# Up-projection operands: made once per pair of tiles, stored to memory and loaded back in two later blocks

## The chip, the cores and the metric

The program runs on one core of a Trainium2 chip. The metric is the device time of one execution in microseconds (us), as a median over runs. The engines are TensorE (PE; its weight loads are listed as PEld), VectorE (DVE), ScalarE (ACT), GpSimd (POOL) and SyncE (SP); each works through its own instruction queue in order and waits on semaphores. Here SP's queue issues nearly all transfers between memory and the on-chip buffers.

## The reference

```python
# attention with decay, per head; state is 64 x 64
state = gamma * state + k_t v_t^T ;  y_t = scale * q_t state
x = y as (3072 tokens, 512)

# first feed-forward layer: 512 -> 2048 -> 512
h = x @ w_in
g = where(h > 0, h, exp(min(h, 0)) - 1)
x = g @ w_out

# second layer: 512 -> 1024 -> 512
h = x @ w_in2 ;  e = exp(h - max(h)) ;  solu = h * e / (sum(e) + 1e-9)
ln = (solu - mean) / sqrt(var + 1e-6) * g_ln
out = ln @ w_out2
```

Every matmul operand is split into a high part, in the format fp32r that PE multiplies, and a low part, the rest (value minus high part). A product is three matmuls: high by high, low by high, high by low.

## The kernel before

There are three stages: attention (to about 82 us of the trace), the first feed-forward layer (to about 570 us), the second layer. The change is in the first layer.

**Blocks and units.** The 3072 tokens are cut in three blocks (`NBLK`) of 1024, and each block in two halves of 512. The 2048 hidden columns are taken 256 at a time: eight units a block (`NFP = 8`), 24 in all (`NU`), numbered n. Unit n of a block multiplies two tiles of `w_in` with both halves of x at once, by Winograd's form of Strassen's product, which needs seven products instead of eight. For that the 2 x 2 arrangement of the weights (A11, A12, A22 and the fourth quadrant, which is loaded into the slot S1) needs four sums (S1 to S4), and x needs four (T1 to T4). The seven left operands, S1 to S4 and three quadrants, each 128 x 256, are the "up operands" of the unit. They depend on the weights and on n % 8, not on the block.

**How the up operands are made.** Two ring slots, n % 2, hold them. Each slot has a high buffer `u_hi` and a low buffer `u_lo`, 7168 bytes a partition each; `u_raw` is another name for the bytes of `u_lo`. For every unit of every block:

- SP, `load_u(n)`: waits until unit n-2 has done its product M4, then loads 512 KB of `w_in` into four of the seven places of `u_raw`.
- POOL, `sum_u(n, i)`, four instructions (L483).
- ACT, `split_u_hi(n)`, one instruction on all seven (L1096), which waits for the fourth sum. It stands in ACT's queue in the middle of `quadrants(n-1)`, ahead of the exponentials of that unit's last three quadrants and ahead of the copy of the next unit's first product (`p1_kept`, L1159).
- POOL, `split_u_lo(n, i)`, seven instructions (L488).
- PE, `up(n, ...)`, lines 618 to 620: waits for `ul_done`, the count of low parts.

**A unit on PE.** `up_pair` runs the products in the order M1, M6, M2, M7, M5, then a `down` product (12 matmuls, L665, L666, L669) of the unit before, then M4 and M3, then the first `down` of this unit: 42 + 24 = 66 matmuls. M2 adds to the bank in which M1 stands, so PE waits for ACT's copy of M1 (`p1_kept`) ahead of it. ACT and DVE make the four quadrants of the hidden values in `quadrants(n)`, with ELU as Relu, Exp and a maximum, and split them into `g_hi` and `g_lo`. After the eight units the second half's 16 `down` products run, in which the next block's x is prepared: DVE's queue holds `sum_x` and `split_x_lo` between its `split_g_lo` instructions (L878), and ACT's queue `split_x_hi` between its `split_g_hi`. The first `sum_x` (L841) stands behind the low split of f = 3 and the evacuation (L884), and ahead of the low split of f = 4; it waits for `load_x`, 2048 KB (L353), which SP issues after product M3 of the block's last unit.

**SP's order around the change.** Attention's loads and the stores of its outputs come first, then 14 loads of `w_out` tiles (`load_wd`, 256 KB each, L364), then the loop over the blocks with `load_u`, the stores of x2 and `load_x`.

The order is written out by hand in each engine's program; no scheduler moves anything.

Of the kernel before, what the change touches and what calls it, by code (L numbers as in the profile page):

```python
# [7 lines left out]
P = 128  # L8
# [18 lines left out]
NFP = NF1 // 2  # L27
NU = NBLK * NFP
# [19 lines left out]
TILE_OF = {place_of(n): n for n in range(NCH)}  # L48


def build(nc, units, w1, w_in2, w_out2, g_ln, tables, x_dram, x2_dram, out):
    f32, f32r = mybir.dt.float32, mybir.dt.float32r
    ALU, ACT, AX = mybir.AluOpType, mybir.ActivationFunctionType, mybir.AxisListType

# [1 line left out]
    with ctx:  # L56
# [8 lines left out]
        def place(name, cols, dt, at):  # L65
            return nc.alloc_sbuf_tensor_at(name, [P, cols], dt, offset=at)
# [40 lines left out]
        u_hi = [place(f"u_hi{s}", 7 * 256, f32r, RING_AT + 14336 * s)[:, :].rearrange("p (o c) -> p o c", c=256)  # L107
                for s in range(2)]
        u_lo = [place(f"u_lo{s}", 7 * 256, f32r, RING_AT + 14336 * s + 7168)[:, :].rearrange("p (o c) -> p o c", c=256)
                for s in range(2)]  # L110
# [89 lines left out]
        def up_bank(blk):  # L200
            return 4 * (blk % 2)
# [11 lines left out]
        def sem(name):  # L213
            return ctx.enter_context(nc.semaphore(name))
# [25 lines left out]
        xh_done = sem("xh_done")  # L240
        xl_done = sem("xl_done")
        u_raw_in = [sem(f"u_raw_in{s}") for s in range(2)]
        u_summed = sem("u_summed")
        uh_done = sem("uh_done")
        ul_done = sem("ul_done")
# [3 lines left out]
        part_done = sem("part_done")  # L249
# [38 lines left out]
        M1, M6, M2, M7, M5, M4, M3 = range(1, 8)  # L288
# [3 lines left out]
        LEFT = [A11, S2, A12, S3, S1, A22, S4]  # L292
# [3 lines left out]
        def products(u, i):  # L296
            return 7 * u + i
# [4 lines left out]
        def quads(n, i):  # L302
            return 4 * n + i

        def after(order, slot):
            return order.index(slot) + 1
# [14 lines left out]
        def _(sp):  # L321
# [29 lines left out]
            def load_x(blk):  # L351
                sp.wait_ge(part_done, products(NFP * blk - 1, M3))
                sp.dma_start(x_raw[:, 0:4, :, :].rearrange("p o k t -> p (o k t)"),  # L353
                             x_dram[blk - 1].rearrange("p h k t -> p (h k t)")).then_inc(x_raw_in, 16)

            def load_u(n):
                if n >= 2:
                    sp.wait_ge(part_done, products(n - 2, M4))
                i = n % NFP
                sp.dma_start(u_raw[n % 2][:, 0:4, :].rearrange("p o c -> p (o c)"),  # L360
                             w1[:, 2 * i:2 * i + 2, :].rearrange("p f c -> p (f c)")).then_inc(u_raw_in[n % 2], 16)

# [3 lines left out]
            def store_x2(blk, half):  # L366
                done = 2 * (2 * blk + half + 1)
                sp.wait_ge(x2_act, done)
                sp.wait_ge(x2_dve, done)
                for i in range(CB):  # L370
                    sp.dma_start(x2_dram[TILE_OF[blk, half, i], :, :].rearrange("p (k t) -> p k t", k=KD),
                                 x2[half][:, :, i * C:(i + 1) * C]).then_inc(x2_stored[half], 16)
# [34 lines left out]
            for blk in range(NBLK):  # L407
                for i in range(NFP):
                    if i == 0 and blk > 0:
                        store_x2(blk - 1, 1)  # L410
                    if NFP * blk + i + 2 < NU:
                        load_u(NFP * blk + i + 2)
                if blk == 0:
                    for s in range(CB, NS):
                        sp.wait_ge(x_stored[s], 32)
                    sp.dma_start(gln_sb[:, :], g_ln).then_inc(gln_in, 16)
                    sp.dma_start(ident[:, :], tables[:, T_IDENT:T_IDENT + P]).then_inc(gln_in, 16)
                if blk < NBLK - 1:
                    load_x(blk + 1)
                    store_x2(blk, 0)  # L420
# [31 lines left out]
        def _(pool):  # L452
# [19 lines left out]
            def sum_u(n, i):  # L472

                raw = u_raw[n % 2]
                to, a, b, op = ((S3, A11, S1, ALU.subtract), (S1, S1, A22, ALU.add),
                                (S2, S1, A11, ALU.subtract), (S4, A12, S2, ALU.subtract))[i]
                if i == 0:
                    pool.wait_ge(u_raw_in[n % 2], 16 * (n // 2 + 1))
                else:
                    pool.wait_ge(u_summed, 4 * n + i)  # L480
                if n >= 2 and to == S4:
                    pool.wait_ge(part_done, products(n - 2, M3))
                nc.gpsimd.tensor_tensor(raw[:, to, :], raw[:, a, :], raw[:, b, :], op).then_inc(u_summed, 1)  # L483

            def split_u_lo(n, i):
                o = LEFT[i]
                pool.wait_ge(uh_done, n + 1)
                nc.gpsimd.tensor_tensor(u_lo[n % 2][:, o, :], u_raw[n % 2][:, o, :], u_hi[n % 2][:, o, :].bitcast(f32),  # L488
                                        ALU.subtract).then_inc(ul_done, 1)
# [3 lines left out]
            for s in range(NS):  # L493
# [6 lines left out]
                if s >= 8:  # L500
                    split_u_lo(0, 2 * (s - 8))
                    if s < NS - 1:
                        split_u_lo(0, 2 * (s - 8) + 1)
            for n in range(1, NU):
                for i in range(4):
                    sum_u(n, i)
                for i in range(7):
                    split_u_lo(n, i)
# [44 lines left out]
        def _(pe):  # L553
# [55 lines left out]

            def up(n, i, bank, a, b, first):  # L610
                blk = n // NFP
                pe.wait_ge(ul_done, products(n, after(LEFT, a)))
                if n % NFP == 0:
                    pe.wait_ge(xl_done, products(blk, after(RIGHT, b)))
                for k in range(2):
                    one = slice(k * P, (k + 1) * P)
                    hi, lo = u_hi[n % 2][:, a, one], u_lo[n % 2][:, a, one]
                    nc.tensor.matmul(bank, hi, x_hi[:, b, k, :], start=(first and k == 0), stop=False, skip_group_check=True)  # L618
                    nc.tensor.matmul(bank, lo, x_hi[:, b, k, :], start=False, stop=False, skip_group_check=True)  # L619
                    done = nc.tensor.matmul(bank, hi, x_lo[:, b, k, :], start=False, stop=(k == 1), skip_group_check=True)  # L620
                done.then_inc(part_done, 1)
# [95 lines left out]
            for blk in range(NBLK):  # L717
                for i in range(NFP):
                    n = NFP * blk + i
# [343 lines left out]
        def _(act):  # L1063
# [61 lines left out]
            def exponent(n, i, h):  # L1125

                z = quads(n, i)
                if z > 3:

                    act.wait_ge(g_done, z - 3)  # L1130
                    if i in (G22, G12):
                        act.wait_ge(gl_done, down_no((n - (i == G22)) // NFP, 0, 2 * ((n - (i == G22)) % NFP) + (i == G22)) + 1)
                one = e[:, (z - 1) % 3, :]
                nc.scalar.activation(one, h, ACT.Relu, scale=-1.0).then_inc(r_done, 1)
                act.wait_ge(r_done, z)
                nc.scalar.activation(one, one, ACT.Exp, scale=-1.0).then_inc(e_done, 1)
# [15 lines left out]
            def quadrants(n):  # L1152
                blk, i = n // NFP, n % NFP
                X = ps[:, up_bank(blk), :]
                e11, e21 = (e[:, (quads(n, q) - 1) % 3, :] for q in (G11, G21))
                act.wait_ge(part_done, products(n, M1))
                if n >= 2:
                    act.wait_ge(g_done, quads(n - 2, G21))
                nc.scalar.activation(p1[:, n % 2, :], X, ACT.Copy).then_inc(p1_kept, 1)  # L1159
                act.wait_ge(part_done, products(n, M2))  # L1160
                exponent(n, G11, X)
                if blk == 0 and i > 0:
                    wd_split_hi(2 * i)
                act.wait_ge(g_done, quads(n, G11))
                split_g_hi(down_no(blk, 0, 2 * i), e11)
                if n + 1 < NU:
                    split_u_hi(n + 1)
                if i == 0 and blk > 0:
                    evacuate(blk - 1, 1)
                if blk == 0 and i > 0:  # L1170
                    wd_split_hi(2 * i + 1)
                act.wait_ge(h_summed, sums(n, H22))
                exponent(n, G22, stash[:, 2 * i + 1, :])
                if i == NFP - 1:
                    split_g_hi(down_no(blk, 1, 0), stash[:, 0, :])
                act.wait_ge(h_summed, sums(n, H21))
                exponent(n, G21, p1[:, n % 2, :])
                act.wait_ge(g_done, quads(n, G21))
                split_g_hi(down_no(blk, 0, 2 * i + 1), e21)
                act.wait_ge(h_summed, sums(n, H12))  # L1180
                exponent(n, G12, stash[:, 2 * i, :])
# [151 lines left out]
```

## Time and profile before

| what | value |
|---|---|
| median of 3 runs | 854.62 us (853.29 to 854.78) |
| profiled execution, own time | 853.04 us |
| its span, first to last instruction | 851.2 us |
| busy: PE / DVE / ACT / POOL | 98% / 64% / 49% / 46% |
| granted TensorE clock, mean | 0.998 |
| memory traffic | 56.50 MB read, 16.78 MB written |
| attention stage ends, unit 0 begins | 82.16 us |

PE's busy share counts pipelined matmuls, whose shown durations (389 ns) overlap; how densely PE works is read from how many matmuls start in a stretch. The other engines' shares are averages over stages. A row of a timeline gives start, duration, engine, line, operation, output and inputs, and in square brackets how long the engine had been idle and what ended that. Rows of SPq are issues of transfers, not the transfers.

### The profile page before, as it was taken

To read this page: it belongs to the slowest core of one execution; us is meant where nothing else is said; L and a number is where in the kernel's file an instruction comes from. 1 tells how busy PE (TensorE), PEld (TensorE's weight loads), DVE (VectorE), ACT (ScalarE), POOL (GpSimd) and SP (SyncE) were. 2 spreads that over 40 slices of the span, in tenths; PEclk is the share of its full clock that TensorE was granted. 3 is DMA by queue.
4 is the path that set the end of the run, shared out by engine and by line. 5 is a ranking of instruction groups with operands and counts; after the bars stand their busy time and mean duration, and the time that the engine had idled before them with its cause. 6 is when DMAs were issued, how large, how long until landed. Compare 5 with 4: busy or idle time off the path is not lost.

```text
span 851.2 us, 12588 instructions
## 1 busy us (share of the span) xinstructions
PE 834.4 (98%) x4850; PEld 691.7 (81%) x4850; DVE 548.3 (64%) x846; ACT 418.5 (49%) x678; POOL 389.2 (46%) x446
## 2 busy tenths in 40 slices
PE   7999999999999999999999999999999999999998
PEld 5888788888888888888888888877888888888886
DVE  2587676768635554575455455787888777777773
ACT  3696656565535555544455554563334333334432
POOL 2669575764016576620267560374253343444200
PEclk9999999999999999999999999999999999999999
DMA  9999610104003010140201002513011111111001
GB/s 348 404 377 313 211 50 25 50 25 170 8 0 99 26 49 26 29 170 1 74 25 50 25 25 87 161 50 99 26 50 50 50 50 38 50 50 50 25 13 50
DMA packets 49643, 74.10 MB, mean 87 GB/s; under 512 B 3248, under 2 KB 23984, under 8 KB 49328
## 3 DMA queue, kind: packets, MB, share of 16 engines
q1 hardware_dynamic: 49152, 73.22, 25.4%
q8 instruction: 39, 0.64, 0.3%
q14 instruction: 20, 0.16, 0.1%
q10 hardware_dynamic: 432, 0.07, 0.0%
HBM read 56.50 MB, written 16.78 MB: 86 GB/s over the span
## 4 chain that ended last, share of the span: by engine, by line
PE 89%; DVE 5%; ACT 2%; POOL 2%; DMA 1%; issue 1%; SPq 0%; DVEq 0%; ACTq 0%
PE ps L665 9%; PE ps L666 9%; PE ps L669 9%; PE ps L618 9%; PE ps L620 9%; PE ps L619 9%; PE ps L766 5%; PE ps L768 5%; PE ps L767 5%; PE ps L677 4%; PE ps L679 4%; PE ps L678 4%; PE ps L595 3%; PE ps L752 2%; PE ps L570 2%; PE ps L583 1%
## 5 line engine op out<-in xcount | busy, mean ns | idle before, releaser
L488 POOL TENSOR_TENSOR u_lo<-u_raw,u_hi 128x256 fp32r<-128x256 f32 x168 | 142.0, 878 | 194.6 <-ACT u_hi L1096 194.6
L665 PE MATMUL ps<-g_hi,wd_hi 128*128 128x512 f32 x384 | 149.4, 389 | 0.0
L666 PE MATMUL ps<-g_hi,wd_lo 128*128 128x512 f32 x384 | 149.4, 389 | 0.0
L669 PE MATMUL ps<-g_lo,wd_hi 128*128 128x512 f32 x384 | 149.4, 389 | 0.0
L618 PE MATMUL ps<-x_hi,u_hi 128*128 128x512 f32 x336 | 131.3, 391 | 0.8 <-ACT p L1159 0.8
L620 PE MATMUL ps<-x_lo,u_hi 128*128 128x512 f32 x336 | 130.8, 389 | 0.0
L619 PE MATMUL ps<-x_hi,u_lo 128*128 128x512 f32 x336 | 130.7, 389 | 0.0
L483 POOL TENSOR_TENSOR u_raw<-u_raw 128x256 f32<-128x256 f32 x96 | 88.0, 917 | 18.0 <-DMA u_raw<-w_dram 12.5
L669 PEld LDWEIGHTS ps<-g_lo,wd_hi 128*128 128x128 f32 x384 | 72.1, 188 | 15.0
L665 PEld LDWEIGHTS ps<-g_hi,wd_hi 128*128 128x128 f32 x384 | 72.1, 188 | 15.0
L666 PEld LDWEIGHTS ps<-g_hi,wd_lo 128*128 128x128 f32 x384 | 72.1, 188 | 14.9
L527 POOL TENSOR_TENSOR u_lo<-x_raw,u_hi 128x256 fp32r<-128x256 f32 x84 | 65.9, 823 | 23.2 <-ACT u_hi L1207 23.2
L766 PE MATMUL ps<-wd_hi,n_hi 128*128 128x512 f32 x192 | 75.8, 395 | 0.0
L618 PEld LDWEIGHTS ps<-x_hi,u_hi 128*128 128x128 f32 x336 | 63.0, 188 | 15.4 <-ACT p L1159 1.9
L768 PE MATMUL ps<-wd_hi,n_lo 128*128 128x512 f32 x192 | 74.8, 389 | 0.0
L767 PE MATMUL ps<-wd_lo,n_hi 128*128 128x512 f32 x192 | 74.8, 389 | 0.0
L620 PEld LDWEIGHTS ps<-x_lo,u_hi 128*128 128x128 f32 x336 | 63.1, 188 | 13.2
L619 PEld LDWEIGHTS ps<-x_hi,u_lo 128*128 128x128 f32 x336 | 63.1, 188 | 13.0
L677 PE MATMUL ps<-x_hi,u_hi 128*128 128x512 f32 x168 | 67.0, 399 | 3.0 <-ACT p L1194 1.8
L533 POOL TENSOR_TENSOR stats<-stats,minus_half 128x1 f32<-128x1 f32 x24 | 13.2, 551 | 115.9 <-DVE stats L999 115.9
L679 PE MATMUL ps<-x_hi,u_lo 128*128 128x512 f32 x168 | 65.6, 391 | 0.0
L678 PE MATMUL ps<-x_lo,u_hi 128*128 128x512 f32 x168 | 65.5, 390 | 0.0
(87 smaller groups left out, 1483.7 us busy)
## 6 DMA issues: line engine op xcount, KB each, us to landing
u_raw<-w_dram SPq DMA_DIRECT2D x24, 512.0 KB, 3.6
k<-units_dram SPq DMA_DIRECT2D x12, 512.0 KB, 8.7
q<-units_dram SPq DMA_DIRECT2D x12, 512.0 KB, 6.1
v<-units_dram SPq DMA_DIRECT2D x12, 512.0 KB, 7.3
x_between<-x SPq DMA_DIRECT2D x24, 256.0 KB, 2.7
x_raw<-x_between SPq DMA_DIRECT2D x12, 512.0 KB, 3.6
out_dram<-y_sb SPq DMA_DIRECT2D x24, 256.0 KB, 2.0
kn<-units_dram SPq DMA_DIRECT2D x10, 512.0 KB, 8.0
```

Source lines behind the costliest of these rows:

```text
L488: nc.gpsimd.tensor_tensor(u_lo[n % 2][:, o, :], u_raw[n % 2][:, o, :], u_hi[n % 2][:, o, :].bitcast(f32), ALU.subtract).then_inc(ul_done, 1)
L618: nc.tensor.matmul(bank, hi, x_hi[:, b, k, :], start=(first and k == 0), stop=False, skip_group_check=True)
L619: nc.tensor.matmul(bank, lo, x_hi[:, b, k, :], start=False, stop=False, skip_group_check=True)
L620: done = nc.tensor.matmul(bank, hi, x_lo[:, b, k, :], start=False, stop=(k == 1), skip_group_check=True)
L665: nc.tensor.matmul(ps[:, bank + m, :], hi, g_hi[:, no % 3, :], start=(f == 0), stop=False)
L666: nc.tensor.matmul(ps[:, bank + m, :], lo, g_hi[:, no % 3, :], start=False, stop=False)
L669: last = nc.tensor.matmul(ps[:, bank + m, :], hi, g_lo[:, no % 3, :], start=False, stop=(f == NF1 - 1))
L677: nc.tensor.matmul(bank, x_h, hi, start=(first and k == 0), stop=False, skip_group_check=True)
L679: done = nc.tensor.matmul(bank, x_l, hi, start=False, stop=(k == 1), skip_group_check=True)
L766: nc.tensor.matmul(bank, n_hi[:, par, f, :], hi, start=(f == 0), stop=False)
L767: nc.tensor.matmul(bank, n_hi[:, par, f, :], lo, start=False, stop=False)
L768: last = nc.tensor.matmul(bank, n_lo[:, par, f, :], hi, start=False, stop=(f == NF2 - 1))
```

## The change

In block 0 the operands are made as before. After each unit's low parts are done, SP's new `store_u(n)` writes both buffers of the slot (2 x 896 KB) to a new internal tensor in memory. For the units of blocks 1 and 2 (n >= 8) `load_u(n)` waits for product M3 of unit n-2 and loads both buffers from there; nothing is summed or split. In block 0 `load_u(n)` for n >= 2 waits in addition for the store of unit n-2, which reads the bytes that it overwrites. In blocks 1 and 2 PE waits once a unit, ahead of M1, for both loads.

```diff
+            def store_u(n):
+
+                sp.wait_ge(ul_done, 7 * (n + 1))
+                for half, part in enumerate((u_hi, u_lo)):
+                    sp.dma_start(u_dram[n, :, half, :, :], part[n % 2].bitcast(f32)).then_inc(u_stored[n % 2], 16)
+
             def load_u(n):
+                i = n % NFP
+                if n >= NFP:
+                    sp.wait_ge(part_done, products(n - 2, M3))
+                    sp.wait_ge(u_stored[n % 2], 32 * (NFP // 2))
+                    for half, part in enumerate((u_hi, u_lo)):
+                        sp.dma_start(part[n % 2].bitcast(f32), u_dram[i, :, half, :, :]).then_inc(u_in[n % 2], 16)
+                    return
                 if n >= 2:
+                    sp.wait_ge(u_stored[n % 2], 32 * (n // 2))
                     sp.wait_ge(part_done, products(n - 2, M4))
-                i = n % NFP
...
+                    if blk == 0:
+                        store_u(i)
                     if NFP * blk + i + 2 < NU:
                         load_u(NFP * blk + i + 2)
...
-            for n in range(1, NU):
+            for n in range(1, NFP):
                 for i in range(4):
                     sum_u(n, i)
                 for i in range(7):
...
-                pe.wait_ge(ul_done, products(n, after(LEFT, a)))
+                if n < NFP:
+                    pe.wait_ge(ul_done, products(n, after(LEFT, a)))
+                elif i == M1:
+                    pe.wait_ge(u_in[n % 2], 32 * ((n - NFP) // 2 + 1))
...
-                if n + 1 < NU:
+                if n + 1 < NFP:
                     split_u_hi(n + 1)
```

SP's queue at the start of block 0, before: the last loads of the `w_out` tiles, then the loads for units 2, 3, 4 and 5 (`u_raw_67` is slot 0, `u_raw_68` slot 1).

```order
L364 DMA wd_raw<-w_dram 128x512 [waits x_stored9,x_stored8,x_stored7]
L364 DMA wd_raw<-w_dram 128x512 x13
L360 DMA u_raw_67<-w_dram 128x1024 [waits part_done]
L360 DMA u_raw_68<-w_dram 128x1024 [waits part_done]
L360 DMA u_raw_67<-w_dram 128x1024 [waits part_done]
L360 DMA u_raw_68<-w_dram 128x1024 [waits part_done]
```

The same place now; `u_between` is the new tensor, `u_hi_63` and `u_lo_65` are slot 0, `u_hi_64` and `u_lo_66` slot 1.

```order
L379 DMA wd_raw<-w_dram 128x512 [waits x_stored9,x_stored8,x_stored7]
L379 DMA wd_raw<-w_dram 128x512 x13
L362 DMA u_between<-u_hi_63 128x1792 [waits ul_done]
L362 DMA u_between<-u_lo_65 128x1792
L375 DMA u_raw_67<-w_dram 128x1024 [waits part_done,u_stored0]
L362 DMA u_between<-u_hi_64 128x1792 [waits ul_done]
L362 DMA u_between<-u_lo_66 128x1792
L375 DMA u_raw_68<-w_dram 128x1024 [waits part_done,u_stored1]
```

Two stores now stand between the `w_out` loads and the load for unit 2, and that load waits for them.

SP's queue at the end of block 0, before: the loads for units 8 and 9, two small tables, and the 2048 KB load of the next block's x.

```order
L360 DMA u_raw_67<-w_dram 128x1024 [waits part_done]
L360 DMA u_raw_68<-w_dram 128x1024 [waits part_done]
L416 DMA gln_sb<-g_ln_dram 128x8 [waits x_stored8,x_stored9,x_stored7,x_stored10,x_stored6,x_stored11,x_stored5,x_stored4]
L417 DMA ident<-tables_dram 128x128
L353 DMA x_raw<-x_between 128x4096 [waits part_done]
L371 DMA x_between<-x_0_79 512x1x128 [waits x2_dve,x2_act]
```

The same place now, from the load for unit 8 on.

```order
L370 DMA u_hi_63<-u_between 128x1792 [waits u_stored0,part_done]
L370 DMA u_lo_65<-u_between 128x1792
L362 DMA u_between<-u_hi_64 128x1792 [waits ul_done]
L362 DMA u_between<-u_lo_66 128x1792
L370 DMA u_hi_64<-u_between 128x1792 [waits u_stored1,part_done]
L370 DMA u_lo_66<-u_between 128x1792
L433 DMA gln_sb<-g_ln_dram 128x8 [waits x_stored8,x_stored9,x_stored7,x_stored10,x_stored6,x_stored11,x_stored5,x_stored4]
L434 DMA ident<-tables_dram 128x128
L355 DMA x_raw<-x_between 128x4096 [waits part_done]
L386 DMA x_between<-x_0_79 512x1x128 [waits x2_dve,x2_act]
```

The load for unit 9 has become two transfers of 896 KB directly ahead of the x load, and it waits for product M3 of the same unit for which the x load waits. At the end of block 1 the same stands there without the stores and the small tables.

## Rows read from the trace of the kernel before

**Rows 1.** Page, part 1: busy time, share, instructions.
```profile
PE 834.4 (98%) x4850; PEld 691.7 (81%) x4850; DVE 548.3 (64%) x846; ACT 418.5 (49%) x678; POOL 389.2 (46%) x446
```

**Rows 2.** Waits of PE, whole span: us in total, times, longest; the first-layer line.
```profile
PE ps L618 <- ACT p L1159: 0.8, 1, 0.8
```

**Rows 3.** Windows: each stretch's busy times, matmul starts in brackets, clock, DMA share, GB/s.
```profile
core 0: us, PE busy (x) PEld busy (x) DVE busy (x) ACT busy (x) POOL busy (x), PEclk, DMA share, GB/s
...
92.00:96.00 4.00, 4.00 (x20) 3.30 (x19) 3.19 (x4) 1.28 (x3) 4.00 (x6) 1.00 1.06 400
...
110.00:150.00 40.00, 40.00 (x178) 33.14 (x177) 27.20 (x36) 25.63 (x39) 24.78 (x28) 1.00 0.10 27
210.00:250.00 40.00, 40.00 (x178) 33.14 (x177) 20.49 (x24) 15.44 (x21) 0.00 (x0) 1.00 0.09 27
...
200.40:205.40 5.00, 5.00 (x23) 4.13 (x22) 4.30 (x5) 2.94 (x5) 4.24 (x5) 1.00 0.93 374
```

**Rows 4.** Timeline of SP's issues at the start of block 0.
```profile
84.45 7.29 SPq L364 DMA_DIRECT2D wd_raw<-w_dram  x14
91.79 0.44 SPq L360 DMA_DIRECT2D u_raw<-w_dram  x1
```

**Rows 5.** Page, part 6: transfers, KB each, median us from issue to landing.
```profile
u_raw<-w_dram SPq DMA_DIRECT2D x24, 512.0 KB, 3.6
...
x_between<-x SPq DMA_DIRECT2D x24, 256.0 KB, 2.7
...
x_raw<-x_between SPq DMA_DIRECT2D x2, 2048.0 KB, 9.4
```

**Rows 6.** Timeline of POOL, units 0 and 1: low splits, sums of unit 2, low splits.
```profile
90.91 5.82 POOL L488 TENSOR_TENSOR u_lo<-u_raw,u_hi 128x256 fp32r<-128x256 f32 x7 [7.05 <-ACT u_hi L1096]
98.34 3.42 POOL L483 TENSOR_TENSOR u_raw<-u_raw 128x256 f32<-128x256 f32 x4 [1.62 <-DMA u_raw<-w_dram]
104.54 6.32 POOL L488 TENSOR_TENSOR u_lo<-u_raw,u_hi 128x256 fp32r<-128x256 f32 x7 [2.78 <-ACT u_hi L1096]
```

**Rows 7.** Timeline of ACT: high split of unit 2 to the copy of M1.
```profile
102.77 1.69 ACT L1096 ACTIVATE u_hi<-u_raw 128x1792 fp32r<-128x1792 f32 x1
...
111.48 0.63 ACT L1136 ACTIVATE e<-e 128x512 f32<-128x512 f32 x1
112.45 0.60 ACT L1159 ACTIVATE p<-ps 128x512 f32<-128x512 f32 x1 [0.34 <-PE ps L620]
```

**Rows 8.** Timeline of PE: last matmul of M6 and first of M2, unit 2.
```profile
113.39 0.39 PE L620 MATMUL ps<-x_lo,u_hi 128*128 128x512 f32 x1
113.61 0.39 PE L618 MATMUL ps<-x_hi,u_hi 128*128 128x512 f32 x1
```

**Rows 9.** Timeline of SP's issues at the end of block 0.
```profile
196.76 0.33 SPq L360 DMA_DIRECT2D u_raw<-w_dram  x1
...
198.25 0.43 SPq L353 DMA_DIRECT2D x_raw<-x_between  x1
```

**Rows 10.** Timeline of DVE at the end of block 0.
```profile
201.87 1.25 DVE L878 TENSOR_TENSOR g_lo<-e,g_hi 128x512 fp32r<-128x512 f32 x1 [0.70 <-ACT g_hi L1145]
...
207.57 1.28 DVE L884 COPY x<-ps 128x512 f32<-128x512 f32 x2
208.76 1.22 DVE L841 TENSOR_TENSOR x_raw<-x_raw 128x1024 f32<-128x1024 f32 x1
209.90 0.69 DVE L878 TENSOR_TENSOR g_lo<-stash,g_hi 128x512 fp32r<-128x512 f32 x1
```

**Rows 11.** Timeline of PE: down product f = 4, its first and third matmul.
```profile
214.25 0.39 PE L665 MATMUL ps<-g_hi,wd_hi 128*128 128x512 f32 x1
214.48 0.39 PE L666 MATMUL ps<-g_hi,wd_lo 128*128 128x512 f32 x1
214.70 0.39 PE L669 MATMUL ps<-g_lo,wd_hi 128*128 128x512 f32 x1
```

**Rows 12.** Timeline of ACT in the first unit of block 1.
```profile
251.01 1.69 ACT L1096 ACTIVATE u_hi<-u_raw 128x1792 fp32r<-128x1792 f32 x1
253.89 1.09 ACT L1150 ACTIVATE x<-ps 128x512 f32<-128x512 f32 x2 [1.20 <-PE ps L669]
```

More of the change, by code:

```diff
@@ L48, with build @@
 TILE_OF = {place_of(n): n for n in range(NCH)}
-def build(nc, units, w1, w_in2, w_out2, g_ln, tables, x_dram, x2_dram, out):
+def build(nc, units, w1, w_in2, w_out2, g_ln, tables, x_dram, u_dram, x2_dram, out):
     f32, f32r = mybir.dt.float32, mybir.dt.float32r
@@ L242, in build @@
         u_raw_in = [sem(f"u_raw_in{s}") for s in range(2)]
+        u_stored = [sem(f"u_stored{s}") for s in range(2)]
+        u_in = [sem(f"u_in{s}") for s in range(2)]
         u_summed = sem("u_summed")
@@ L1327 @@
     args.append(nc.dram_tensor("x_between", (NBLK - 1, P, 2, KD, TB), mybir.dt.float32, kind="Internal").ap())
+    args.append(nc.dram_tensor("u_between", (NFP, P, 2, 7, 256), mybir.dt.float32, kind="Internal").ap())
     args.append(nc.dram_tensor("x2_between", (NT, P, KD * P), mybir.dt.float32, kind="Internal").ap())
```

## The prediction

> **What bounds the kernel now.** I read the page's busy line first, then PE's waits, then how densely PE starts matmuls, and only then the queues around the change. PE is busy 98% of the span, POOL 46%, ACT 49% [rows 1]; so work taken from POOL and ACT is worth only what PE waits for it. In the whole first layer PE has one listed wait, 0.8 us, for ACT [rows 2]. Because shown durations overlap, the better test is the count: 178 matmuls start in 40 us while POOL is 62% busy (24.78 of 40), and 178 in 40 us while POOL does nothing [rows 3]. That is 0.2247 us a matmul both times (a few records may be missing), at clock 1.00. The layer runs at PE's own pace, and POOL's work does not slow it. The reader is to see that nearly nothing is left to gain, and that the question is which cover the new transfers use up.
>
> **What is removed.** 16 of 24 units lose four sums and seven low splits on POOL and one high split on ACT: 3.42 + 6.32 + 1.69 us a unit [rows 6, 7], about 183 us of engine time. All of it lies beside PE's work. I also looked at the one place in blocks 1 and 2 where ACT's split could be late, the first unit of a block: the split at 251.01 ends at 252.7, and ACT then idles 1.20 us until PE has finished the product that the evacuation needs [rows 12]. Without the split ACT idles about 2.9 us and the evacuation starts at the same 253.89. Gain: 0. PE's 16 x 6 waits fewer for low parts cost nothing that the count of matmuls shows. Value of the removal: 0, from 0 to 0.4 us.
>
> DVE does get faster. A low split takes 1.25 us beside POOL and 0.69 us when POOL idles [rows 10]. The Trainium skill (SBUF — State Buffer, "Who interferes with whom") says that a DVE instruction with two on-chip inputs contends with a GpSimd instruction that reads the same memory; the row agrees. By that rule the change relieves DVE in 16 units, and if PE waited for DVE there it would be worth a rival, below.
>
> **What is added at the start of block 0.** This is the term that decides. Before, SP issues 14 loads of 256 KB from 84.45 to 91.74 and then the load for unit 2 at 91.79 [rows 4]. The transfers are behind the issues: from 92 to 96 the engines move 400 GB/s at a full share [rows 3]. The load for unit 2 lands as POOL starts its sums, 98.34 [rows 6], 6.5 us after its issue, where a load of this size takes 3.6 us otherwise [rows 5]. So it waited behind the weights.
>
> Now the store of unit 0, whose low parts have long been made, is issued in this place (two issues of 0.44 us, still under the backlog), and the load for unit 2 waits until it has landed:
>
> - The store is 2 x 896 KB = 1.835 MB, the old load 0.524 MB. At 400 GB/s it lands (1.835 - 0.524)/400 = 3.3 us after the old load did, at 101.6. With the slope between the 512 KB and the 2048 KB load (9.4 - 3.6 us for 1536 KB, 3.8 ns a KB) [rows 5] the extra 1280 KB cost 4.8 us: 103.1. Large writes are not in the trace; a 256 KB one takes 2.7 us [rows 5], so writes are not plainly slower. The stream at 400 GB/s is the nearer row, as here too the queue is full; I take 101.8.
> - SP issues the load for unit 2: +0.1, and 3.6 us to landing [rows 5]: 105.5.
> - Four sums: 3.42 us before [rows 6], in part beside DVE; now DVE is idle for part of it. I take 3.1: 108.6.
> - ACT's high split of unit 2 stood at 102.77, one us after the sums ended at 101.76. It can start at 108.7, 5.9 us late. ACT's queue is blocked by it: behind it stand the exponentials of three quadrants of unit 1, and DVE waits for those. The chain from there to ACT being free again took 102.77 to 112.11 (111.48 + 0.63) [rows 7], with POOL's low splits beside it as they will be again, so it moves as a whole.
> - Cover: ACT had 0.34 us to spare ahead of the copy of M1 [rows 7]; that copy ended at 113.05 and M2 began at 113.61 [rows 8], so PE had another 0.5. Cover 0.84. Stall ahead of M2 of unit 2: 5.9 - 0.8 = 5.1 us.
>
> The bounds: everything at the fast end (101.6, sums 3.0) gives 4.8; the slope and 3.4 us of sums give 6.7. PE also waits about 0.5 us for the first low part ahead of M1; that lies inside the same stall.
>
> Next is unit 3. The store of unit 1 follows the load for unit 2 and lands near 110.5, so the load for unit 3 is issued then and not at 106.8, lands at 114.1, and its sums come after POOL's low splits of unit 2 anyway (110.4 to 116.7), ending at 120.5. ACT wants them 14.96 us after its place for unit 2 (one unit is 66 matmuls of 0.2267 us), plus the stall: 122.8. Hidden, by 2.3 us. From then on a unit's low splits end at 110.86 + 14.96 x k; its store needs 6.6 to 8.4 us, and the load that waits for it is due 10.8 us after the splits end. Hidden by 2 to 4 us, and the sums behind it have some 6 us more. So the stall comes once, not eight times.
>
> **What is added at the ends of blocks 0 and 1.** The x load was issued at 198.25 [rows 9] and takes 9.4 us [rows 5]; DVE takes it up at 208.76, behind its evacuation [rows 10]. Now the load for unit 9 moves from 196.76 to 198.1 (it waits for M3) and is 1.835 MB; the x load is issued at 199.8 and queues behind it. Data from 200.1: 1.835/400 = 4.7 us, then 2.097 MB at 374 GB/s [rows 3], 5.6 us, and the last pieces straggled 1.3 us before: it lands at 211.7. DVE's queue has the first sum of x ahead of the low split of f = 4. That split ended at 210.59, and PE wants it for the third matmul of that product, 214.70 [rows 10, 11]. With 1.9 us for sum and split and 0.1 to wake, x may land at 212.7. Hidden with 1.0 us to spare; at the end of block 1, with no small tables between, with 1.8. ACT's queue has more room. If it fails: if the straggling doubles with the bytes the landing is 213.0 and the stall 0.3 us; at the slope's rate for all of it 217 and 4 us. I cost it 0.
>
> **The two loads a unit in blocks 1 and 2** are issued after M3 of unit n-2, and land in 7 to 9 us; one unit later, 14.96 us and a down product, PE wants them. Hidden. So is the store of unit 7: it lands near 194, ahead of 198. Memory traffic rises by 14.7 MB written and 21 MB read (16 x 1.835 instead of 16 x 0.524), all in the stretches at 27 GB/s [rows 3].
>
> **Sum.** +5.1 on the one path, 0 elsewhere. On the profiled execution's own time, 853.04 (span 851.2 and 1.84 around it), that is 858.1; the median of the three runs lies 1.58 above that execution, which gives 859.7. The mean of all four times is 853.9; I forecast 859.0.
>
> **Rivals.**
>
> *B, the seams give way too.* As above, but the x load lands after 212.7 in both blocks and DVE's low splits hold PE. For it: 1.0 us of room only, and stragglers in the x load. Against: DVE needs 1.8 us per f where PE needs 2.72, so it catches up at once. Price 1 to 2 us each: 862.
>
> *C, the stores are slow.* If large writes run at half the rate, 200 GB/s, the store of unit 0 takes 9.2 us instead of 4.6 and the stall is 9.6: 863.5. Against: the 256 KB write's 2.7 us. The Trainium skill (DMA: Bandwidth & Descriptors, the bandwidth table at its head) gives memory a limit of 358 GB/s per core; the stream of 400 GB/s in the row is above that, and by the page the store would take 5.1 us and the sum would be 0.5 higher.
>
> *D, no change.* If the store lands by 97 or so, or the block of ACT's queue is absorbed before M2, nothing shows: 853.9. For it: the store is issued with half the backlog drained. Against: the store is 3.5 times the transfer that itself landed at 98.3, and cover is 0.84 us.
>
> *E, faster.* The place is each unit of blocks 1 and 2, the mechanism DVE relieved of POOL: 0.56 us (1.25 - 0.69) less per unit, if PE waited for that split. 16 x 0.56 = 9 us: 850 with the stall, 845 without. It decides from the point where PE waits for DVE by more than nothing in a unit. Against: PE's only wait is for ACT, and the two counts of 178 are equal [rows 2, 3].
>
> **How the numbers follow.** Forecast A, one stall of 4.8 to 6.7: 0.62, own range 857.5 to 861.5 with the runs' spread. B 0.12, C 0.12, D 0.10, E 0.04. The range 856.8 to 863.6 takes in A, B and the near side of C. Within 0.2% (1.7 us, about what a measurement can tell from no change) is D, 0.10; faster E, 0.04, less what is left of it with the stall, 0.03; slower A, B, C: 0.87.
>
> **What would show it.** In the new profile: the load for unit 2 issued near 101.9 instead of 91.8; POOL's sums near 105.5; ACT's split near 108.7; one wait of PE of about 5 us ahead of M2 of unit 2, and from there block 1 in step with before, shifted by it; POOL idle from unit 8 on; DVE's splits at 0.69 us. I am wrong if PE waits again in units 3 to 7 (stores slower than taken), if it waits in the down products f = 4 or 5 of the second half (B), or if matmuls in blocks 1 and 2 start less densely than 178 in 40 us, which would mean that 1.835 MB a unit disturb PE.

## The result

| | before | after |
|---|---|---|
| median of 4 runs | 853.95 us (853.13 to 854.78) | 860.36 us (859.77 to 862.11) |
| ratio, 95% interval | | 1.007 [1.0052, 1.0088] |
| profiled execution / span | 853.04 / 851.2 us | 860.7 / 858.9 us |
| POOL busy | 389.2 us | 238.8 us |
| ACT busy | 418.5 us | 394.5 us |
| memory read / written | 56.50 / 16.78 MB | 77.48 / 31.46 MB |

The changed kernel is 0.7% slower, +6.4 us by the medians; the forecast was 859.0. POOL lost 150 us of work and nothing came of it.

The profile after, in the order of the prediction's steps. SP's issues at the start of block 0 (start, us, then the transfer; to be read beside [rows 4]):

```profile
84.78 7.21 SPq L379 DMA_DIRECT2D wd_raw<-w_dram  x14
92.04 0.47 SPq L362 DMA_DIRECT2D u_between<-u_hi  x1
92.56 0.43 SPq L362 DMA_DIRECT2D u_between<-u_lo  x1
101.85 0.33 SPq L375 DMA_DIRECT2D u_raw<-w_dram  x1
102.23 0.44 SPq L362 DMA_DIRECT2D u_between<-u_hi  x1
102.71 0.43 SPq L362 DMA_DIRECT2D u_between<-u_lo  x1
110.83 0.33 SPq L375 DMA_DIRECT2D u_raw<-w_dram  x1
```

The load for unit 2 is issued 10.1 us later than before. POOL follows it [rows 6]:

```profile
106.58 3.19 POOL L500 TENSOR_TENSOR u_raw<-u_raw 128x256 f32<-128x256 f32 x4 [9.52 <-DMA u_raw<-w_dram]
111.58 6.22 POOL L505 TENSOR_TENSOR u_lo<-u_raw,u_hi 128x256 fp32r<-128x256 f32 x7 [1.81 <-ACT u_hi L1116]
```

ACT, whose split at 102.77 had no idle time ahead of it [rows 7], now stands still for it with everything queued behind:

```profile
102.56 0.64 ACT L1165 ACTIVATE g_hi<-e 128x512 fp32r<-128x512 f32 x1 [0.23 <-DVE e L893]
109.81 1.70 ACT L1116 ACTIVATE u_hi<-u_raw 128x1792 fp32r<-128x1792 f32 x1 [6.61 <-POOL u_raw L500]
...
118.43 0.63 ACT L1156 ACTIVATE e<-e 128x512 f32<-128x512 f32 x1
118.97 0.58 ACT L1179 ACTIVATE p<-ps 128x512 f32<-128x512 f32 x1
```

PE, the first matmuls of M2 of unit 2 (before: no gap, [rows 8]):

```profile
119.60 0.50 PE L638 MATMUL ps<-x_hi,u_hi 128*128 128x512 f32 x1 [3.27 <-ACT p L1179]
119.94 0.40 PE L639 MATMUL ps<-x_hi,u_lo 128*128 128x512 f32 x1
120.17 0.47 PE L640 MATMUL ps<-x_lo,u_hi 128*128 128x512 f32 x1
120.44 0.63 PE L638 MATMUL ps<-x_hi,u_hi 128*128 128x512 f32 x1
120.87 0.63 PE L639 MATMUL ps<-x_hi,u_lo 128*128 128x512 f32 x1
121.30 0.63 PE L640 MATMUL ps<-x_lo,u_hi 128*128 128x512 f32 x1
```

PE's listed waits from unit 0 to unit 2 (window 84 to 130 us; of the first line 0.8 us are in unit 1, as before [rows 2], and 3.3 ahead of M2):

```profile
PE ps L638 <- ACT p L1179: 4.1, 2, 3.3
PE ps L638 <- POOL u_lo L505: 1.1, 1, 1.1
PE ps L638 <- DVE p L888: 0.6, 1, 0.6
```

The stall is where it was put, but it is three waits and not one: 1.1 us ahead of M1 for the first low part, 0.6 us ahead of M6 for a sum of DVE in unit 1's quadrants, and 3.3 us ahead of M2 for ACT's copy. All three stand behind ACT's late split. What was not forecast stands in the last rows of the timeline: matmuls start 0.427 us apart instead of 0.227. The windows show the granted clock (0.61 on average, 12 matmuls in 4.4 us), and that blocks 1 and 2 keep PE's pace, with 138 GB/s of loads and POOL idle (compare 178 in 40 us, [rows 3]). The number in brackets counts every matmul that a window touches, also those under way at its start: the 178 of before are 176 starts, 0.227 us apart, and not 0.2247 as the prediction has it. The comparison of two such windows stands all the same. The windows:

```profile
98.85:119.60 20.75, 15.84 (x66) 12.15 (x66) 9.60 (x14) 9.29 (x14) 10.90 (x13) 1.00 0.56 206
119.60:124.00 4.40, 4.40 (x12) 3.50 (x13) 1.92 (x4) 1.78 (x4) 1.81 (x3) 0.61 0.75 314
...
277.00:317.00 40.00, 40.00 (x179) 33.10 (x178) 18.96 (x28) 17.89 (x30) 0.00 (x0) 1.00 0.37 138
```

DVE at the end of block 0, shifted by 7.8 us against [rows 10]:

```profile
215.34 1.28 DVE L904 COPY x<-ps 128x512 f32<-128x512 f32 x2
218.95 1.23 DVE L861 TENSOR_TENSOR x_raw<-x_raw 128x1024 f32<-128x1024 f32 x1 [2.33 <-DMA x_raw<-x_between]
220.10 0.69 DVE L898 TENSOR_TENSOR g_lo<-stash,g_hi 128x512 fp32r<-128x512 f32 x1
```

DVE now waits 2.33 us for x; PE does not wait: from behind the slow matmuls to the second layer no two matmuls start more than 0.35 us apart, the end of block 1 included.

### The profile page after: what moved, and what is told of

Same layout as the page of the kernel before. It is cut to its first block, busy times and chain, and to the rows that moved or that the text cites. A ratio compares the mean times of both kernels' runs of the same rounds, so it can differ in the third digit from the quotient of the medians.

```text
span 858.9 us, 12346 instructions
## 1 busy us (share of the span) xinstructions
PE 836.1 (97%) x4850; PEld 692.4 (81%) x4850; DVE 539.9 (63%) x846; ACT 394.5 (46%) x662; POOL 238.8 (28%) x270
## 3 DMA queue, kind: packets, MB, share of 16 engines
HBM read 77.48 MB, written 31.46 MB: 127 GB/s over the span
## 4 chain that ended last, share of the span: by engine, by line
PE 86%; DVE 5%; DMA 3%; POOL 2%; ACT 2%; issue 1%; SPq 1%; ACTq 0%; DVEq 0%; POOLq 0%
PE ps L686 9%; PE ps L689 9%; PE ps L685 9%; PE ps L638 8%; PE ps L639 8%; PE ps L640 8%; PE ps L786 5%; PE ps L787 5%; PE ps L788 5%; PE ps L697 4%; PE ps L699 4%; PE ps L698 4%; PE ps L612 2%; PE ps L772 2%; PE ps L587 2%
## 5 line engine op out<-in xcount | busy, mean ns | idle before, releaser
L530 POOL TENSOR_TENSOR x_raw<-x_raw 128x256 f32<-128x256 f32 x12 | 10.4, 865 | 388.9 <-DMA x_raw<-x_between 388.9
L1156 ACT ACTIVATE e<-e 128x512 f32<-128x512 f32 x96 | 60.7, 632 | 3.1
L1244 ACT ACTIVATE n_hi<-ps 128x512 fp32r<-128x512 f32 x48 | 26.1, 595 | 70.3 <-PE ps L772 70.3
```

## The experiments

The time of a whole run varies by 2 to 4 us, largely in the attention stage, in which the edits change nothing: unit 0 begins anywhere from 81.74 to 86.50 us in the traces below. A finer measure is the *layer*: from the start of unit 0's first matmul to the last matmul ahead of the 2.18 us gap in the opening of the second layer. Its value is 485.94 us in the trace before (82.16 to 568.10), and three of the kernels below agree with that within 0.02. Its two ends in the trace before:

```profile
82.16 0.50 PE L618 MATMUL ps<-x_hi,u_hi 128*128 128x512 f32 x1
...
568.10 0.39 PE L679 MATMUL ps<-x_hi,u_lo 128*128 128x512 f32 x1
570.29 0.50 PE L677 MATMUL ps<-x_hi,u_hi 128*128 128x512 f32 x1 [1.80 <-ACT p L1194]
```

Each trace is one execution. "ACT late" is the start of the high split of unit 2 counted from the start of unit 0, less that before (102.77 - 82.16). "Low clock" is how long the granted clock stood at 0.5 in block 0, in us. The control is the changed kernel again, run in one session with "stores only, again" and "extra matmuls in three gaps".

| kernel | ratio to before, 95% | ACT late | layer, from and to | layer - before | low clock |
|---|---|---|---|---|---|
| changed | 1.007 [1.0052, 1.0088] | 6.70 | 82.50, 575.83 | +7.39 | 3.41 |
| changed, again | 1.0068 [1.0047, 1.0089] | 6.24 | 83.82, 575.03 | +5.27 | 0 |
| no store of unit 0 | 1.0004 [0.9992, 1.0016] | 0.04 | 83.40, 569.34 | 0.00 | 0 |
| loads only | 1.0007 [0.9998, 1.0016] | -0.01 | 81.74, 567.68 | 0.00 | 0 |
| stores only | 1.0093 [1.0077, 1.011] | 5.94 | 86.50, 577.44 | +5.01 | 0 |
| stores only, again | 1.0089 [1.0066, 1.0113] | 6.02 | 83.63, 576.12 | +6.55 | 3.41 |
| store 0 before the weights | 1.0032 [1.0019, 1.0045] | 3.44 | 83.58, 572.12 | +2.61 | 0 |
| reordered | 0.999 [0.9976, 1.0005] | 0.01 | 81.94, 567.90 | +0.02 | 0 |
| store 1 held | 1.007 [1.0051, 1.0089] | 5.36 | 81.87, 575.15 | +7.34 | 6.83 |
| extra matmuls ahead of M2 | 1.0063 [1.0051, 1.0075] | 6.49 | 82.33, 573.84 | +5.57 | 0 |
| extra matmuls in three gaps | 1.0072 [1.0049, 1.0094] | 6.80 | 83.24, 575.10 | +5.92 | 0 |

**No store of unit 0.**

```diff
                 if n >= 2:
-                    sp.wait_ge(u_stored[n % 2], 32 * (n // 2))
+                    if n != 2:
+                        sp.wait_ge(u_stored[n % 2], 32 * ((n - 1) // 2))
...
-                    if blk == 0:
+                    if blk == 0 and i > 0:
                         store_u(i)
```

> Leaves out: the store of unit 0's operands; units 8 and 16 load unit 1's instead. So the load for unit 2 waits for product M4 of unit 0 alone, as in the kernel before. Theory (T), one store: the store of unit 0 costs everything, by way of the load for unit 2, ACT's queue and the lower clock behind PE's idle time. Expected: no idle of PE ahead of M2 of unit 2, clock 1.00 through block 0, 854.0 us, ratio to before 0.999 to 1.001. Rival (R), traffic: seven stores and 32 loads remain, so if the bytes themselves disturb PE or the queues, 7/8 of the loss remains, 859.5 us.

854.71 us against 854.35, and the layer took 485.94 us, as before. PE's only listed wait in it is the one that before had:

```profile
PE ps L639 <- ACT p L1180: 0.8, 1, 0.8
```

Seven stores and 32 loads remain in it. Their bytes cost nothing; one store out of eight costs everything. The rival of traffic is out.

**Loads only.**

```diff
                 if n >= 2:
-                    sp.wait_ge(u_stored[n % 2], 32 * (n // 2))
...
-                    if blk == 0:
+                    if blk == 0 and i == NFP - 2:
                         store_u(i)
...
-                        sp.dma_start(part[n % 2].bitcast(f32), u_dram[i, :, half, :, :])
+                        sp.dma_start(part[n % 2].bitcast(f32), u_dram[NFP - 2, :, half, :, :])
```

> Leaves out: the stores of units 0 to 5 and 7; every unit of blocks 1 and 2 loads unit 6's operands (2 x 896 KB each, as in the change). The load for unit 2 waits for M4 of unit 0 alone. T: 854.0 us, ratio 0.999 to 1.001: loads hidden, POOL's relief worth 0. R2: below 853 if the relief is worth more than 1 us. R: above 855 if the loads disturb, above all the x load at the ends of blocks 0 and 1, which still stands behind 1.835 MB.

854.84 against 854.35, layer 485.94. The half of the change that relieves POOL and ACT is worth 0, with the x load behind 1.835 MB as in the change.

**Stores only,** run in two sessions.

```diff
-            for n in range(1, NFP):
+            for n in range(1, NU):
                 for i in range(4):
                     sum_u(n, i)
...
-                if n + 1 < NFP:
+                if n + 1 < NU:
                     split_u_hi(n + 1)
```

> All eight stores with their waits, but the operands of blocks 1 and 2 are made anew as in the kernel before; nothing is loaded back. T: the loss is in the stores' half of the change and the other half is worth nothing, so 860.4 us (859.7 to 861.1). R2, a hidden gain: if taking the making of operands off POOL and ACT gained something that the stores' loss covers, this kernel is slower than the changed one by that gain, 1 us or more, 861.5 us.

> The kernel with stores only once more. In its first trace the first layer, from PE's gap in unit 1 to its gap at the start of the second layer, took 475.8 us with the clock at 1.00, 2.4 less than in the changed kernel, whose clock fell there; what made the run longer lay in the attention stage, which the edit does not touch. T: same time as the changed kernel within the intervals, and the layer 5.6 to 7.4 us above before depending on the clock. R2, a hidden gain of POOL's relief: 1 us or more slower than the control.

862.29 and 861.92 us, where the changed kernel had 860.30 in the second session. The layer says that stores alone make the whole stall (+5.01 with the clock up, +6.55 with one fall; the changed kernel +5.27 and +7.39), so no gain of POOL's relief is hidden there. But the run times are 1.6 to 1.9 us above the changed kernel's (860.36 and 860.30), more than T allowed and what R2 asked for; only the layer speaks against R2, and the intervals of the ratios overlap. In the first trace the excess is not in the layer: attention ended 4.0 us later than in the changed kernel's trace (86.50 against 82.50), with the granted clock at 0.5 for 3.41 us from 76.7. The mean granted clocks of these runs are lower (0.990 to 0.998, mostly 0.994 to 0.996; the control five times 0.998 and once 0.994), and 3.41 us at half clock are 0.002 of the mean. At an equal mean clock of 0.996 the two kernels are close: five runs with stores only average 861.2 us, three of the changed kernel's first four 860.9. So more time at the low clock fits part of the excess; whether this kernel really has more of it, and why, was not found. This stays open.

**The changed kernel again.**

> The changed kernel itself, as a control in the same session as the next two. 860.4 us, ratio to before 1.007.

860.30 us. Its trace is the most useful one: the same gap of PE, and the clock did not fall. First the wait, then the window behind it:

```profile
120.49 0.51 PE L638 MATMUL ps<-x_hi,u_hi 128*128 128x512 f32 x1 [3.28 <-ACT p L1179]
```

```profile
120.50:124.50 4.00, 4.00 (x18) 3.31 (x19) 2.18 (x4) 2.06 (x4) 1.81 (x3) 1.00 0.82 344
```

17 matmuls start in these 4 us, with the transfers as dense as in the first trace: what slowed PE there was the clock and not the stores' traffic.

**Store of unit 0 ahead of the weight loads.**

```diff
+            store_u(0)
             for f in range(2, NF1):
                 load_wd(f)
...
-                    if blk == 0:
+                    if blk == 0 and i > 0:
                         store_u(i)
```

> The store of unit 0 is issued ahead of the 14 weight loads instead of behind them. T with a full queue: the store lands early, so the load for unit 2 is issued at about 92.5 again, but it still stands behind 4.6 us more of data and lands near 103, not 98.3; ACT's split is 3.6 us late instead of 6.7, the stall 2.8 us, and the result 856.7 us, or 858 if the clock falls all the same. Rival, only the wait counts: with the wait met early the stall is gone, 854.0 us.

857.57 us, 2.6 above before in its session. POOL and ACT in this trace (unit 0 begins at 83.58):

```profile
103.89 3.71 POOL L501 TENSOR_TENSOR u_raw<-u_raw 128x256 f32<-128x256 f32 x4 [5.73 <-DMA u_raw<-w_dram]
...
107.63 1.71 ACT L1117 ACTIVATE u_hi<-u_raw 128x1792 fp32r<-128x1792 f32 x1 [3.34 <-POOL u_raw L501]
```

ACT is 3.4 us late, the layer 2.61 longer, 2.8 expected. So the wait on the store is only part of it: the load also pays for the bytes ahead of it. One detail was missed: the load was issued at 96.36 and not at 92.5, because SP's 14 weight issues took 9.34 us behind the store, where they take 7.2.

**Reordered:** the same, and the last eight weight loads behind the load for unit 2.

```diff
+            store_u(0)
-            for f in range(2, NF1):
+            for f in range(2, 8):
                 load_wd(f)
...
                         load_u(NFP * blk + i + 2)
+                    if blk == 0 and i == 0:
+                        for f in range(8, NF1):
+                            load_wd(f)
```

> As before it, and the last 8 of the 14 weight loads are issued behind the load for unit 2 (the first of them is needed by unit 4, about 35 us later). T: the load for unit 2 lands by 98, no stall, 854.0 us, ratio to before 0.999 to 1.001. R: other stores and loads disturb, 855 us or more. Nobody expects less than 853: PE works without a gap in the layer, so there is nothing for POOL's relief to give.

854.06 against 854.95 us, no difference that can be told; all eight stores and all loads are in it.

```profile
97.19 3.53 POOL L504 TENSOR_TENSOR u_raw<-u_raw 128x256 f32<-128x256 f32 x4 [0.67 <-DMA u_raw<-w_dram]
...
102.56 1.69 ACT L1120 ACTIVATE u_hi<-u_raw 128x1792 fp32r<-128x1792 f32 x1
112.24 0.60 ACT L1183 ACTIVATE p<-ps 128x512 f32<-128x512 f32 x1 [0.33 <-PE ps L644]
```

ACT's split is back in its place without idle time, and ACT has its 0.33 us to spare again. The idea of the change costs nothing when its first store is out of the way, and gains nothing either.

**Store of unit 1 held back.**

```diff
                 sp.wait_ge(ul_done, 7 * (n + 1))
+                if n == 1:
+                    sp.wait_ge(u_raw_in[0], 32)
```

> The changed kernel, but SP holds the store of unit 1 until the load for unit 2 has landed. In the changed kernel that load took 4.7 us instead of 3.6, with the store of unit 1 issued right behind it. If the two shared the engines, the load takes 3.6 us again and the stall is 1.1 us shorter: 859.3 us. If the load was slow for another reason, nothing changes: 860.4 us. The load for unit 3 goes out some 3 us later, which POOL's low splits of unit 2 still cover.

The time did not move: 861.11 us, not the 859.3 expected, the interval that of the changed kernel. The mechanism did: the load was issued at 101.16 and POOL began at 104.63, 3.5 us later, where the changed kernel's two traces had 4.7 and 4.3.

```profile
101.16 0.33 SPq L377 DMA_DIRECT2D u_raw<-w_dram  x1
104.62 0.32 SPq L364 DMA_DIRECT2D u_between<-u_hi  x1
```

ACT was 5.36 us late instead of 6.24 to 6.70. In this trace the clock then stood low for 6.83 us, some 14 matmuls each 0.2 us further from the next, 2.9 us, which hides the 0.9 to 1.3 us won. With that taken off the layer is +4.4.

**Extra matmuls in PE's gaps.** The second version has the lines ahead of M1 (5) and M6 (3) as well.

```diff
                 up(n, M6, Y, S2, T2, True)
+                if n == 2:
+                    for _ in range(15):
+                        nc.tensor.matmul(ps[:, 3, :], u_hi[0][:, A11, 0:P], x_hi[:, B11, 0, :], start=True, stop=True)
                 pe.wait_ge(p1_kept, n + 1)
```

> The changed kernel with 15 extra matmuls of 512 columns into a bank that nobody reads, ahead of PE's wait for the copy of M1 in unit 2, where PE idled 3.4 us. They start 0.227 us apart, 3.4 us in all, so M2 starts when it did. Theory (C), clock: the 8 or so matmuls that followed 0.427 us apart at granted clock 0.5 were slow because PE had stood idle; with PE kept at work the clock stays at 1.00 and 1.6 us come back: 858.8 us. Rival: the slow stretch has another cause (the stores' traffic at that time); then it stays and the extra matmuls cost 0 to 0.3 us: 860.4 to 860.7 us.

> Extra matmuls in all three gaps of PE around unit 2: 5 ahead of M1, 3 ahead of M6, 15 ahead of M2. C: PE is not idle for longer than 1 us anywhere near, the clock stays at 1.00 through block 0, the stall stays; layer 5.6 us above before, time 1 to 1.6 us below the control. Rival: the clock falls at the same place though PE is at work, time as the control.

859.37 and 861.16 us; the control 860.30. Neither can be told from it, and the gain of 1 to 1.6 us that the second was to bring did not come. M2 started no earlier: the layer, +5.57 and +5.92, is what ACT's lateness makes it (6.49 and 6.80, less the 0.84 us of cover, are 5.65 and 5.96). In both traces the clock stayed at 1.00 in block 0, but so it did in two of the five traces with the open gap. This fits the theory that idle time brings the clock down, but does not show it, and it does not show that filling is worth anything.

## Why the prediction was right

- *The removal is worth 0.* Right: loads only and reordered have the layer of before. DVE's low splits are at 0.69 us beside an idle POOL, and PE did not want them earlier. They gained less than the 0.56 us a unit that the prediction gave rival E, because most of them were not slowed before either. One of the two groups, over 150 us of blocks 1 and 2, before (262 to 412) and after (270 to 420); behind the bar stand the busy us, then the mean ns of one:

```profile
L878 DVE TENSOR_TENSOR g_lo<-stash,g_hi 128x512 fp32r<-128x512 f32 x16 | 12.0, 758 | 12.2 <-ACT g_hi L1145 12.2
L898 DVE TENSOR_TENSOR g_lo<-stash,g_hi 128x512 fp32r<-128x512 f32 x16 | 11.1, 692 | 12.9 <-ACT g_hi L1165 12.9
```

- *The store of unit 0 delays the load for unit 2.* The load was to be issued at 101.9; counted from unit 0 (0.33 later in this trace) it went out at 101.5. The bound of 3.8 ns a KB was too slow, the full queue's 400 GB/s the right row.
- *3.6 us to landing.* This term of the sum was too small: 4.7 and 4.3, because the store of unit 1, which SP issues 0.4 us behind, takes part of the engines. Held back, it was 3.5. The prediction had the transfers come strictly one after another. The 0.4 us of the early issue hides part of this error.
- *Sums 3.1 us.* 3.19.
- *Cover 0.84.* ACT late less 0.84 gives 5.86, 5.40, 4.52 and 2.60 for the changed kernel, its repeat, store 1 held and store 0 first; measured, with 1.6 and 2.9 us for the low clock taken off: 5.8, 5.3, 4.4 and 2.6. Stores only gives 5.10 where 5.01 was measured. This is the step on which the stall's size hangs, and it holds over the whole range.
- *One wait of about 5 us ahead of M2.* Right in its size and its cause, not in its form: three waits, 1.1, 0.6 and 3.3 us. The prediction had named the first, at 0.5 us, and not the second.
- *Once, not eight times.* Right: behind unit 2's slow matmuls no two starts of PE are more than 0.35 us apart until the second layer. The load for unit 3 was issued at 110.83 (forecast: 110.5), and ACT took up its split at 124.51 without idle time.
- *x load at the block ends.* Landing forecast 211.7, shifted by 7.8 is 219.5; it was 218.9, 1.6 us ahead of the limit. Rival B did not happen.
- *Rival C* (slow stores) is out: the eight 896 KB stores of the high parts land in 3.6 us (median). The limit of 358 GB/s per core that the Trainium skill gives (DMA: Bandwidth & Descriptors, the bandwidth table at its head) would by estimate have added 0.5 us. The trace does not bear it out here: the load was issued 0.4 us earlier than forecast, and from 96.0 to 98.3 us the engines moved 439 GB/s. *D* is out: the store let the load for unit 2 go 10.1 us later, and the cover was 0.84 us. *E* failed where it was said to: PE waits for DVE nowhere in blocks 1 and 2.
- *Not forecast:* the clock. In the first trace the stall was 5.8 us and the clock fell, 1.6 us more: 8 matmuls 0.2 us further apart. The median's +6.4 lies between the +5.3 and +7.4 of the two traces. The size was thus 1.3 us short. ACT's later split accounts for 0.3 to 0.8 of it; that the rest is the clock, in some runs and not in others, is argued from two traces and not shown run by run.

## What to carry to other kernels

Ahead of taking work off an engine, ask what PE waits for; here it was 0.8 us in the whole layer, and equal counts of matmuls per 40 us showed it. What the new transfers cost here was decided where their queue was already full and the cover thinnest: eight equal stores, and only the first mattered, by 5.3 to 5.8 us without the clock, because a prefetch waited behind it and one engine's in-order queue turned a late buffer into a late everything. Moving eight loads that nobody needed yet behind the urgent one took the whole loss back.

## What was not expected of the hardware

In the layer and behind it the granted clock fell to half (2.4 to 1.2 GHz) around gaps of PE, from 0.6 us ahead of PE's next matmul to 0.8 us behind it. It stayed there for 3.41 us or 6.83, and it did not fall every time. A gap of 3.7 us between two starts in unit 2 went with a fall in three of five traces. The 2.18 us gap at the opening of the second layer, which every kernel has, went without one in eight of twelve traces, before and the changed kernel among them, and with one in loads only, reordered, store 1 held and extra matmuls in three gaps. What decides it these runs do not show. The window of the first of these four, in which 8 matmuls start in 3.4 us:

```profile
570.70:574.10 3.40, 3.40 (x10) 2.62 (x9) 1.12 (x2) 0.60 (x1) 3.40 (x5) 0.51 0.00 0
```

Such a fall costs 1.6 us in block 0. At the opening of the second layer it costs about 1.2 us: from the end of the layer to the end of the span it is 283.1 to 283.5 us in the eight traces without it, 284.2 to 284.9 in the four with it. That is as much as the differences in question; the layer's length with the clock read beside it settled most of what medians of 4 to 12 runs did not.
